# Retention and two feed-forward layers on one core: LayerNorm's turn by VectorE squares and transfers from GpSimd

## What is computed

```python
def _moe2_ref(x, w_in, w_out, g_ln):        # x: 3072 x 512, w_in: 512 x 1024, w_out: 1024 x 512
    h = x @ w_in
    e = np.exp(h - np.max(h, axis=-1, keepdims=True))
    sm = e / (np.sum(e, axis=-1, keepdims=True) + 1e-09)
    solu = h * sm
    mu = np.mean(solu, axis=-1, keepdims=True)
    var = np.mean((solu - mu) ** 2, axis=-1, keepdims=True)
    ln = (solu - mu) / np.sqrt(var + 1e-06) * g_ln
    return (ln @ w_out).astype(np.float32)
```

## Time and profile before

| | us |
|---|---|
| median of 3 runs | 980.58 (980.35 to 981.1) |
| the profiled execution | 983.99 |
| its span in the profile | 982.2, granted clock 0.997 |

### The profile page before, as it was taken

One profiled execution on the slowest core, in us unless ns is written; L12 is line 12 of the kernel. 1 busy time (PEld: TensorE's weight loads), 2 busy tenths in 40 slices (PEclk: granted clock), 3 DMA queues, 4 the chain that ended last, 5 costly groups with the idle time before them and its releaser, 6 DMA issues.

```text
span 982.2 us, 15207 instructions
## 1 busy us (share of the span) xinstructions
PE 958.3 (98%) x5494; PEld 849.6 (86%) x5494; DVE 616.8 (63%) x1054; ACT 548.3 (56%) x940; POOL 135.5 (14%) x170
## 2 busy tenths in 40 slices
PE   8879899999999999999999999999999999999998
PEld 4666787887899999999999999999888888888887
DVE  3777886777778653544678877677554444544442
ACT  3554645555465442433445555554687776667765
POOL 4313401102015510000151101010000000000000
PEclk9989999999999999999999999999999999999999
DMA  8747636536143513131553735521411111111100
GB/s 264 226 138 213 185 134 184 171 141 185 54 182 113 193 49 114 65 113 57 174 200 117 242 116 179 178 81 43 161 44 43 43 43 43 43 43 43 46 29 33
DMA packets 82320, 116.03 MB, mean 118 GB/s; under 512 B 7120, under 2 KB 62800, under 8 KB 82256
## 3 DMA queue, kind: packets, MB, share of 16 engines
q1 hardware_dynamic: 76800, 98.79, 30.6%
q0 software_dynamic: 4736, 15.73, 4.6%
q10 hardware_dynamic: 720, 0.66, 0.2%
HBM read 77.41 MB, written 37.75 MB: 117 GB/s over the span
## 4 chain that ended last, share of the span: by engine, by line
PE 83%; DVE 5%; issue 3%; DMA 3%; ACT 2%; POOL 2%; SPq 1%; DVEq 0%; ACTq 0%; POOLq 0%
PE psum L884 10%; PE psum L887 10%; PE psum L886 10%; PE psum L359 9%; PE psum L361 9%; PE psum L360 9%; PE psum L922 6%; PE psum L920 6%; PE psum L923 6%; PE psum L777 3%; PE psum L811 2%; PE psum L964 2%; PE psum L801 2%; PE psum L790 2%; DMA w_raw<-weights 1%
## 5 line engine op out<-in xcount | busy, mean ns | idle before, releaser
L884 PE MATMUL psum<-xo_hi,w_hi 128*128 128x384 f32 x560 | 195.3, 349 | 6.7 <-DVE psum L1494 2.6
L887 PE MATMUL psum<-xo_hi,w_lo 128*128 128x384 f32 x560 | 188.4, 336 | 0.0
L886 PE MATMUL psum<-xo_lo,w_hi 128*128 128x384 f32 x560 | 188.3, 336 | 0.0
L884 PEld LDWEIGHTS psum<-xo_hi,w_hi 128*128 128x128 f32 x560 | 105.9, 189 | 13.1 <-DVE xo_lo L1480 3.8
L886 PEld LDWEIGHTS psum<-xo_lo,w_hi 128*128 128x128 f32 x560 | 105.9, 189 | 0.8 <-issue 0.3
L1102 ACT ACTIVATE xo_hi<-b 128x768 fp32r<-128x768 f32 x84 | 70.6, 846 | 63.6 <-PE psum L923 51.9
L887 PEld LDWEIGHTS psum<-xo_hi,w_lo 128*128 128x128 f32 x560 | 105.7, 189 | 0.0
L1374 DVE TENSOR_TENSOR xo_lo<-b,xo_hi 128x768 fp32r<-128x768 f32 x84 | 80.0, 955 | 34.3 <-ACT xo_hi L1102 34.0
L359 PE MATMUL psum<-w_in_hi,x_hi 128*128 128x512 f32 x192 | 76.8, 400 | 0.3 <-ACT h_buf L1223 0.3
L361 PE MATMUL psum<-w_in_hi,x_lo 128*128 128x512 f32 x192 | 74.9, 390 | 0.0
L360 PE MATMUL psum<-w_in_lo,x_hi 128*128 128x512 f32 x192 | 74.9, 390 | 0.0
(11 more groups left out here) (128 smaller groups left out, 2065.8 us busy)
## 6 DMA issues: line engine op xcount, KB each, us to landing
act_dram<-act_buf SPq DMA_DIRECT2D x48, 384.0 KB, 2.4
b<-act_dram SPq DMA_DIRECT2D x48, 384.0 KB, 4.8
kq_buf<-k_t SPq DMA_DIRECT2D x32, 192.0 KB, 2.7
kq_buf<-q_t SPq DMA_DIRECT2D x64, 96.0 KB, 3.0
q_dec<-q_t SPq DMA_DIRECT2D x32, 192.0 KB, 2.5
w_raw<-weights POOLq DMA_DIRECT2D x12, 512.0 KB, 4.6
x_dram<-x_tile SPq DMA_DIRECT2D x4, 1536.0 KB, 6.0
x_tile<-x_dram SPq DMA_DIRECT2D x4, 1536.0 KB, 6.8
```

Source lines behind the costliest of these rows:

```text
L884: pe.matmul(dst, hi[:, cols], xo_hi[:, i, kc, :], start=i in (P1, P7) and kc == 0, stop=False, skip_group_check=True)
L886: pe.matmul(dst, hi[:, cols], xo_lo[:, i, kc, :], start=False, stop=False, skip_group_check=True)
L887: mm = pe.matmul(dst, lo[:, cols], xo_hi[:, i, kc, :], start=False, stop=kc == HK - 1, skip_group_check=True)
```

## The change

Tile 0 is turned as before. For tiles 1 to 5 there is no `turn` on PE:

- DVE, `normalize`: (solu - mean) * rstd in one instruction, in place; the mean is made negative by `negative_mean`, and the deviation must be known first: ACT squares with the mean as bias (`square_solu`) and takes the root for two blocks at a time (`deviation_of_pair`), DVE inverts both (`invert_pair`).
- DVE, `turn_blocks`: one instruction turns each 32 x 32 square of the block's 128 x 1024 and writes the squares to `z`, one of two buffers of a whole tile.
- POOL, `move_turned`: 16 transfers per tile, each from 32 partitions to 32 partitions of `ln_t`, 128 KB in pieces of 512 B. Four of them (f = 0 to 3) make slice i of `ln_t`. A slice holds 32 tokens of each of the tile's four blocks, so every transfer waits for all four turned blocks of the tile, and for `ln_low` of the slice that it overwrites.
- ACT's `ln_high` and DVE's `ln_low` read the slice from SBUF; ACT waits for its four transfers. `scale_out` has no scale any more. `store_out` writes four groups of 32 rows, 128 rows apart, in place of 128 rows in a row.
- As the turned tile is needed whole, the blocks' ups run six ahead of the down2 in place of two: tile 0 has ten ups beside four down2, and no ups are left after down2(4, 0).
- All tiles are written out; there is no loop. `load_x2` runs two tiles ahead.

```diff
-            def stage_c(t, first, last):          # PE
+            def stage_c(t):
+                if t == 0:
...
+                    both_down2(0, 0)
+                    both_up(0, 3)
+                    for j in range(1, BLOCKS):
+                        turn(0, j)
+                        both_up((2 * j + 2) // BLOCKS, (2 * j + 2) % BLOCKS)
+                        both_down2(0, j)
+                        both_up((2 * j + 3) // BLOCKS, (2 * j + 3) % BLOCKS)
+                    return
                 for j in range(BLOCKS):
...
-                        turn(t, j)
...
+                    if run_up_of(t, j):
+                        both_up(*run_up_of(t, j))
+                    both_down2(t, j)

+        def run_up_of(t, j):
+            tile, block = (t + 1, j + 2) if j < 2 else (t + 2, j - 2)
+            return (tile, block) if tile < C_TILES else None

+            def normalize(t, j):                  # DVE
+                dve.wait_ge(pair_rstd_ready, 2 * (t - 1) + j // 2 + 1)
+                dve.tensor_scalar(solu[:, j % 2, :], solu[:, j % 2, :], mean[:, j:j + 1], rstd[:, j:j + 1], ALU.add,
+                                  ALU.mult).then_inc(normalized, 1)
+            def turn_blocks(t, j):
+                n = t * BLOCKS + j
+                dve.wait_ge(normalized, n - BLOCKS + 1)
+                if j == 0:
+                    for i in range(PARTS):
+                        at_least(dve, ln_t_moved[i], DMA * PARTS * (t - 2))
+                dve.transpose(z_of(t)[:, :, :, j, :].rearrange("p k f c -> p (k f) c"),
+                              solu[:, j % 2, :].rearrange("p (b r) -> p b r", r=32)).then_inc(z_ready, 1)

+            def move_turned(t):                   # POOL
+                for i in range(PARTS):
+                    pool.wait_ge(z_ready, BLOCKS * t)
+                    pool.wait_ge(ln_lo_ready, 2 * (BLOCKS * (t - 1) + i + 1))
+                    for f in range(PARTS):
+                        pool.dma_start(ln_t[32 * f:32 * f + 32, i, :, :],
+                                     z_of(t)[32 * i:32 * i + 32, :, f, :, :].rearrange("p k j c -> p k (j c)")).then_inc(
+                                         ln_t_moved[i], DMA)

                 for j in range(BLOCKS):           # ACT, tiles 1 to 5
...
+                    if j > 0:
+                        scale_out(t, j - 1)
+                    elif t > 1:
                         scale_out(t - 1, 3)
                     ln_high(t, j, 0)
                     ln_high(t, j, 1)
...
+                    last_up = (t + 1, j + 1) if j < 3 else (t + 2, 0)
+                    if last_up[0] < C_TILES:
+                        square_solu(*last_up)
+                        if j % 2 == 0:
+                            deviation_of_pair(t + 1, j // 2)
+                    if run_up_of(t, j):
+                        copy_h(*run_up_of(t, j), 0)
+                        if j % 2 == 1 and t + 2 < C_TILES:
+                            x2_high(t + 2, j // 2)
+                        copy_h(*run_up_of(t, j), 1)
+                        exponent(*run_up_of(t, j))

                 for j in range(BLOCKS):           # DVE, tiles 1 to 5
+                    both_low(t, j)
+                    if t + 1 < C_TILES:
+                        if j % 2 == 0:
+                            invert_pair(t + 1, j // 2)
+                        turn_up(t + 1, j)
+                    if run_up_of(t, j):
+                        row_max(*run_up_of(t, j))
+                        if j % 2 == 1 and t + 2 < C_TILES:
+                            x2_low(t + 2, j // 2)
+                        take_up(*run_up_of(t, j))

+                    deviation_of_pair(1, 1)       # ACT, tile 0, towards its end
+                    deviation(0, 3)
+                    copy_h(2, 0, 1)
+                    exponent(2, 0)
+                    x2_high(2, 1)
+                    scale_out(0, 3)
+                    copy_h(2, 1, 0)
+                    square_solu(2, 0)
+                    copy_h(2, 1, 1)
+                    exponent(2, 1)

+                    turn_up(1, 3)                 # DVE, tile 0, its last lines
+                    x2_low(2, 1)
+                    invert_deviation(0, 3)
+                    take_up(2, 0)
+                    row_max(2, 1)
+                    take_up(2, 1)

+                if t == 0:                        # store_out, SP
+                    rows = out[n * P:(n + 1) * P, :]
+                else:
+                    rows = out[bass.ds(t * TC, TC), :].rearrange("(b i c) d -> i b c d", b=BLOCKS, i=PARTS)[j]
```

More of the change, by code:

```diff
@@ L321, in retention_moe_kernel @@
         squares_summed = sem("squares_summed")
+        d_squared = sem("d_squared")
+        pair_std_ready = sem("pair_std_ready")
+        pair_rstd_ready = sem("pair_rstd_ready")
+        normalized = sem("normalized")
+        z_ready = sem("z_ready")
+        ln_t_moved = [sem(f"ln_t_moved{i}") for i in range(PARTS)]
         std_ready = sem("std_ready")
@@ L336, in x_bank, with tiles, solu_of, z_of @@
             return SUM if n == 1 else PX
[L338 to L345, removed]
+        def tiles(step):
+            for t in range(C_TILES):
+                step(t)
+        def run_up_of(t, j):
+            tile, block = (t + 1, j + 2) if j < 2 else (t + 2, j - 2)
+            return (tile, block) if tile < C_TILES else None
+        def solu_of(t, j):
+            return solu_0[:, j, :] if t == 0 else solu[:, j % 2, :]
+        def z_of(t):
+            return z1 if t % 2 else z0
         def windows(attention_step, point):
@@ L640, in _ @@
             load_x2(1, 0)
+            load_x2(0, 1)
             for k in range(6, F2C):
@@ L1027, in _ @@
+            tiles(stage_c)
         @block.scalar
@@ L1286, in stage_c @@
                 for j in range(BLOCKS):
-                    start = first and j == 0
-                    if start:
-                        copy_h(t, 2, 0)
-                    elif j == 0:
+                    if j > 0:
+                        scale_out(t, j - 1)
+                    elif t > 1:
                         scale_out(t - 1, 3)
-                    elif not last or j < 2:
-                        scale_out(t, j - 1)
                     ln_high(t, j, 0)
                     ln_high(t, j, 1)
-                    if start:
-                        exponent(t, 1)
@@ L1298, in stage_c @@
-                    deviation(t, j)
-                    if last and j >= 2:
-                        scale_out(t, j - 1)
-                        continue
-                    nt, nj = (t, j + 2) if j < 2 else (t + 1, j - 2)
-                    if not start:
-                        copy_h(nt, nj, 0)
-                    if not last and j in (0, 2):
-                        x2_high(t + 1, j // 2)
-                    copy_h(nt, nj, 1)
-                    exponent(nt, nj)
-            tiles(act, stage_c)
+                    last_up = (t + 1, j + 1) if j < 3 else (t + 2, 0)
@@ L1570, in softmax_h @@
                 dve.wait_ge(sum_inverted, n + 1)
-                dve.scalar_tensor_tensor(out=solu[:, j % 2, :], in0=h_buf[:, j % 2, :], scalar=e_inv[:, one],
+                if n == 0:
+                    for s in range(4):
+                        dve.wait_ge(x2_stored[s], DMA * 2 * B)
+                dve.scalar_tensor_tensor(out=solu_of(t, j), in0=h_buf[:, j % 2, :], scalar=e_inv[:, one],
                                          in1=e_buf[:, j % 2, :], op0=ALU.mult, op1=ALU.mult,
```

265 lines of the change are left out of this document (183 added, 82 removed).

## The result

The changed kernel took 993.5 us (median of 4 runs, 992.8 to 996.26), the kernel before on the same chip 980.84 (980.35 to 982.83): a ratio of 1.013, 95% interval 1.0106 to 1.0155. The forecast was 984.2 with a range of 979.5 to 992.0. The direction was right; the size was not: +12.7 in place of +3.6. The changed kernel, timed once more beside the last experiments, gave 1.011 (1.0093 to 1.0128).

A forecast was written before the change was run, and what follows sets the result against it. TensorE (PE) was taken as the bound; -17.8 for turns, +3.8, +10.5 and +4.7 for waits, +0.9 restarts and +1.5 store summed to +3.6 us on 980.58, so 984.2 us, range 979.5 to 992.

The forecast's parts named there:

- turns gone: Tiles 1 to 5 lose their turns on PE: 20 blocks at 0.89 us each, -17.8 us.
- boundary 0-1: From tile 0 to 1, PE waits 1.8 us ahead of up(2,2) and then 2.0 us: together +3.8 us.
- five direct successions: In the tail, down2 following down2 at (4,2), (4,3), (5,1), (5,2), (5,3) waits 2.1 us each through ACT's order: +10.5 us.
- (5,0): First down2 of tile 5 waits for turn, four transfer issues, landing, ln_high and ln_low: +4.7 us.
- restarts: PE's first step after each of eight waits takes 0.11 us longer: +0.9 us.
- clock in the tail: PE's clock falling in waits: nothing in the sum; ten slow steps behind the longest wait, 2.3 us, inside the range.
- last store: The final output store, writing 4 groups of 32 rows, is exposed: +1.5 us, between 0 and +2.4.
- rival 1: Tile boundaries don't bind; only the six direct down2 successions in the tail cost: -4.5 us, 976.1 us; chance 15%.
- rival 2: POOL's issues or the landing are slow, so boundaries 1-2, 2-3 and 3-4 wait too: +18.2, about 1002 us; 13%.
- Rival 3: DVE's square turn takes two passes, 1.07 us more each: +4.5, 988.7 us; chance 10%.
- Rival 4: DVE's normalize keeps POOL from issuing transfers: changes the sum by under 0.8, 985 us; chance 2%.
- Rival 5: PE's clock falls in the waits, a step 0.227 us longer; ten steps, 2.3 us, inside the range; no chance given.

The follow-up runs named there:

- after_again: The changed kernel timed and profiled once more, unedited; ratio to the kernel before 1.011 (1.0093 to 1.0128).
- after: The changed kernel as first measured and profiled; median 993.5 us, ratio to the kernel before 1.013.
- first_order: The changed kernel with tile 0's hand-written orders on ACT and DVE rearranged; ratio to the kernel before 1.008.
- tail_order: The changed kernel with ACT doing ln_high ahead of the previous block's scale_out for five blocks of the tail; ratio to the kernel before 0.9996.
- squares_1_to_4_sp: The changed kernel with tile 5 turned by PE, tile 0 and tail orders mended, last tile's rows stored plainly, moves on SP; 0.9857 of the kernel before.

## Why the prediction was wrong, step by step

| step | predicted | measured |
|---|---|---|
| turns gone | -17.8 | -17.7 (20 turns of 0.885, by the starts in the trace before) |
| boundary 0-1 | +3.8 | +4.2 (2.48 and 1.73); the second by a chain that the working left out as well |
| five direct successions | +10.5 | +10.5 (5 x 2.09) |
| (5,0) | +4.7 | +3.9 |
| restarts | +0.9 | +1.1 |
| clock in the tail | 0 in the sum, 2.3 in the range | +4.1 (19 slow steps 3.8, the steps in which it changed 0.3); 26 slow steps, 5.2, in after_again |
| last store | +1.5, at most 2.4 | +3.7 |
| a wait at the start of the stage | nothing | +1.0: 1.4 lost in after (1.27 idle ahead of 700.51), 0.4 before, none in after_again; profiles of both kernels have it or not |
| sum | +3.6 | +10.8 |

Right, and shown by rows or experiments: the first wait at 0-1 and the five of the tail come from the orders alone (first_order, tail_order), the steady boundaries are hidden, the square turn is one pass, (5,0) has its chain. On (5,0) the working was close (D is the start of down2(4,3)): z complete at D+2.6 (2.4 predicted), POOL starts 0.3 later, four issues 2.3 (3.0), landing 3.0 (3.5).

Near by its number, and in part by luck: the second wait at 0-1. The prediction put it down to DVE's order alone and wrote against rival 1 that neither wait at 0-1 contains a transfer. In the trace the moved slice comes at the same moment, 8.1 us after POOL's first issue (775.22 to 783.34) where the prediction's four issues and landing are 6.5. Mending the order left 1.09 of it, and moves from SP on top of that 0.28 (squares_1_to_4_sp). So the landing behind POOL is a bound there, as rival 2 had it, though not at the steady boundaries.

On the rivals as they stood: rival 1 is refuted, since (5,0) and the boundary 0-1 bind. Rival 2 is refuted as a whole by the boundaries 1-2, 2-3 and 3-4, which have no wait. Rival 3 is refuted by 1246 ns for the turn. Rival 4 was not put to the test: no normalize ran beside any of the 80 issues (one batch is issued from 817.0 to 826.2, the next normalize starts at 827.83), so their 582 to 610 ns say nothing on it; it could cost nothing here.

The step that failed is the size of two terms of the sum, +0 for the clock and +1.5 for the last store. They are 6.3 of the 7.2 us by which the profile's +10.8 exceeds +3.6; the wait at the start of the stage is 1.0, and the others nearly cancel. Against the first median, +12.7, another 1.9 stay unassigned.

*The last store.* "At most +2.4" came from scaling its bytes by four along. But fewer engines is not more bytes. Before, 0.7 us at 301 GB/s carried most of it (211 of 262 KB); after, the first of the three microseconds shown moves only 29 GB/s at a share of 0.24, and the third 100. The Trainium skill, "DMA: Bandwidth & Descriptors", "Why a DMA increments its semaphore by 16 and not by 1", gives 4 engines for this shape; the trace agrees (share 0.24 to 0.26). The estimate of +1.7 from its bandwidth was too low too, by 2.0. What fills the slow first part no run here takes apart.

*The clock.* Rival 5 had the mechanism and nearly the price of a step (0.227 for 0.200 measured); it had ten slow steps behind the longest wait. There were 12 behind (5,0), and 7 more in a second stretch behind waits of 1.93, which I had not counted on: 19 in all, and 26 in the other profile's tail. It also stood without a chance and outside the sum, "inside the range", though the forecast itself had PE standing still six times in 50 us. A consequence that follows from the forecast's own waits belongs in its sum. With 4.1 and 3.7 in place of 0 and 1.5 the sum is +9.9, 990.5.

The range's high end (992) was built from the uncertainty of the turn and the issues, which turned out near or below the value taken. What widened the time was in the two other terms.

## What to carry to other kernels

Where a change takes work off the bound engine but leaves its last items following each other directly, write the tail's order anew: here 10.5 us of waits came from an order (copy out, then prepare the next) that was harmless as long as other work lay between, and the tail's waits (14.4 us with (5,0)) then cost 4 to 5 us more in clock. If part of the work does not hide, do that part the old way: turning the last tile on PE cost 3.6 us and saved the long wait, the slow clock and the divided store. And before an output is permuted on its way out, look at the slowest dimension of the transfer: nothing hid the last store here. And a wait that an order explains can have a second chain that ends close behind it, as at down2(1,0); mending the order then gives back only the difference.

## What the runs showed of the hardware

- The granted clock fell to 0.50 not only behind a wait of 3.75 us but also in rows of waits of 1.93 us with 5.5 us of matmuls between them (after, 970 to 975), behind the first wait of 1.93 after a long unbroken stretch (after_again, 934 to 937), and behind a wait of 2.3 (after_again, 777 to 780). Which of the waits it follows differs from one execution to the next; the number of slow steps was 19 and 34 for one kernel. Behind (5,0) matmuls of 0.23 us a step ran at 0.43 for 5.7 us. Useless matmuls in the waits of the tail kept it at 1.00 there.
- With a last 256 KB store of 4 x 32 rows of 2 KB the span ended 6.3 us after its issue, and it moved at up to 100 GB/s; with 128 rows in a row the span ended 2.5 us after the issue (979.72 to 982.2), 0.7 us of it at 301 GB/s. Its issue on SP took 0.53 for 0.33.
- SBUF-to-SBUF transfers of 128 KB in 256 pieces of 512 B: POOL issued one in 0.58 us, SP in 0.62 (median); in batches of 16 they landed in 6.1 from POOL and 3.0 from SP. Loads of x (512 KB) beside them took 7.9 with POOL's moves, 5.4 with SP's.
- VectorE turned 128 x 1024 f32 in 32 x 32 squares in 1.25 us; a reduction over as much took 1.22.
